# Chunks of tokens that never cross a batch edge, in an attention woven into a two-layer MLP kernel

## The reference

```python
k_p = k.reshape(B, H, 72, 8, D).mean(axis=3)
v_p = v.reshape(B, H, 72, 8, D).mean(axis=3)
scores = scale * np.matmul(q, k_p.transpose(0, 1, 3, 2))
scores = scores - np.max(scores, axis=-1, keepdims=True)
attn = np.exp(scores)
attn = attn / (np.sum(attn, axis=-1, keepdims=True) + 1e-09)
x = np.matmul(attn, v_p)                    # -> 4608 tokens x 512
# layer 1: h = x @ w_in; g = h if h >= 1, 0 if h <= -1, else (h + 1)**2 / 4; x = g @ w_out
# layer 2: h = x @ w_in; g = h - tanh(h);                                    x = g @ w_out
```

## Time and profile before

| | |
|---|---|
| median of 3 runs | 1709.42 us (1708.79 to 1709.98) |
| the profiled execution's own time | 1709.42 us |
| its span in the trace | 1707.7 us |
| PE busy | 1677.3 us, 98% |
| DVE / ACT / POOL busy | 768.4 / 496.2 / 183.9 us |
| mean DMA rate | 46 GB/s |

### The profile page before, as it was taken

How to read it: one execution, slowest core, us unless ns; L and a number is a source line. 1 busy time by engine, 2 the same in 40 slices (tenths; PEclk the granted TensorE clock), 3 DMA queues, 4 the chain that set the end, 5 groups by cost and what they waited for, 6 DMA issues and landing times.

```text
span 1707.7 us, 17885 instructions
## 1 busy us (share of the span) xinstructions
PE 1677.3 (98%) x7668; PEld 1392.3 (82%) x7668; DVE 768.4 (45%) x1197; ACT 496.2 (29%) x816; POOL 183.9 (11%) x133
## 2 busy tenths in 40 slices
PE   4999999999999999999999999999999999999998
PEld 3888888888888888888888888888888888888887
DVE  7666656575665647555443323222232323232322
ACT  3533232323333233232343222222222222222221
POOL 4730202020020202001044000000000000000000
PEclk8999999999999999999999999999999999999999
DMA  9102011110201121010223010101010101010000
GB/s 314 62 28 86 29 50 38 53 62 29 86 28 50 37 78 38 0 50 1 74 99 124 0 50 1 50 0 50 0 50 0 50 0 50 1 50 1 25 1 25
DMA packets 40208, 77.71 MB, mean 46 GB/s; under 512 B 3264, under 2 KB 3264, under 8 KB 40128
## 3 DMA queue, kind: packets, MB, share of 16 engines
q1 hardware_dynamic: 40128, 76.56, 13.3%
HBM read 57.67 MB, written 18.87 MB: 45 GB/s over the span
## 4 chain that ended last, share of the span: by engine, by line
PE 98%; POOL 1%; SPq 1%; DMA 0%; DVE 0%; issue 0%; ACT 0%; POOLq 0%
PE acc_ps L453 46%; PE h_ps L445 33%; PE att_ps L445 7%; PE score_ps L445 6%; PE score_ps L490 1%; PE att_ps L469 1%; PE score_ps L469 1%; PE att_ps L481 1%; PE att_ps L490 0%; PE score_ps L491 0%; SPq L284 0%; DMA v_raw<-v 0%; POOL v_raw L391 0%; POOL prob L413 0%; PE score_ps L481 0%; PE att_ps L491 0%
## 5 line engine op out<-in xcount | busy, mean ns | idle before, releaser
L453 PE MATMUL acc_ps<-g_hi,wout_hi 128*128 128x512 f32 x1152 | 454.2, 394 | 0.0
L453 PE MATMUL acc_ps<-g_hi,wout_lo 128*128 128x512 f32 x1152 | 449.0, 390 | 0.0
L453 PE MATMUL acc_ps<-g_lo,wout_hi 128*128 128x512 f32 x1152 | 448.8, 390 | 0.0
L445 PE MATMUL h_ps<-x_hi,win_hi 128*128 128x512 f32 x828 | 328.7, 397 | 1.4 <-DVE x_lo L816 1.4
L445 PE MATMUL h_ps<-x_hi,win_lo 128*128 128x512 f32 x828 | 322.9, 390 | 0.0
L445 PE MATMUL h_ps<-x_lo,win_hi 128*128 128x512 f32 x828 | 322.6, 390 | 0.0
L730 DVE TENSOR_TENSOR h_ps<-h_ps,bent 128x512 f32<-128x512 f32 x207 | 144.5, 698 | 272.1 <-ACT bent L603 206.1
L453 PEld LDWEIGHTS acc_ps<-g_hi,wout_lo 128*128 128x128 f32 x1152 | 216.2, 188 | 46.1
L453 PEld LDWEIGHTS acc_ps<-g_hi,wout_hi 128*128 128x128 f32 x1152 | 216.3, 188 | 43.9 <-issue 0.8
L453 PEld LDWEIGHTS acc_ps<-g_lo,wout_hi 128*128 128x128 f32 x1152 | 216.6, 188 | 43.4
L719 DVE TENSOR_TENSOR g_lo<-h_ps,g_hi 128x512 fp32r<-128x512 f32 x207 | 143.0, 691 | 125.6 <-ACT g_hi L607 124.9
(11 more groups left out here) (128 smaller groups left out, 1488.5 us busy)
## 6 DMA issues: line engine op xcount, KB each, us to landing
stage<-kT SPq DMA_DIRECT2D x16, 576.0 KB, 4.9
q_sb<-qT SPq DMA_DIRECT2D x9, 1024.0 KB, 5.1
x2T_scratch<-out_sb SPq DMA_DIRECT2D x9, 1024.0 KB, 4.1
x_lo<-x2T_scratch SPq DMA_DIRECT2D x9, 1024.0 KB, 7.3
yT<-out_sb SPq DMA_DIRECT2D x9, 1024.0 KB, 5.1
win_raw<-w_in SPq DMA_DIRECT2D x8, 1024.0 KB, 6.0
wout_raw<-w_out SPq DMA_DIRECT2D x8, 1024.0 KB, 7.8
stage<-v SPq DMA_DIRECT2D x7, 1024.0 KB, 5.8
```

The costliest lines, as they stand in the source:

```text
L445: last = nc.tensor.matmul(h_bank(j, layer), w[:, c, j * P:(j + 1) * P], x_[:, c, :], start=(c == 0 and i == 0), stop=(c == KT - 1 and i == 2))
L453: last = nc.tensor.matmul(acc_ps[:, m, :], w[:, j, m * P:(m + 1) * P], g[:, j % GRING, :], start=(j == 0 and i == 0), stop=(j == FT - 1 an ...
```

## The change

`chunks(n)` now returns a flat list of (first column, rows, batch). A chunk that the edge would cut becomes two chunks of 64 rows. So n = 1, 3, 5, 7 have five chunks, two of them with 64 rows, and ten units at steps 2 to 6; the other n have four chunks of 128 as before. Every half has its own scores (to PSUM rows 0 to 63), maximum, shift, exponential, sum, reciprocal, normalisation, and its own transposes in each turn, with 64 weight rows, 64 moving columns of the identity, and 64 columns of the output bank. `CHMAX` goes from 4 to 5, so `prob` and the arena are 576 words longer, only chunks from the second on can lie under `out_sb`, and the wait for the store moves from chunk 0 to chunk 1.

```diff
-CHMAX = T // P
+CHMAX = 5
...
     for c in range(T // P):
-        cut = min(max(edge - c * P, 0), P)
-        out.append([part for part in [(0, cut, n - 1), (cut, P - cut, n)] if part[1] > 0])
+        lo, hi = c * P, (c + 1) * P
+        if hi <= edge:
+            out.append((lo, P, n - 1))
+        elif lo >= edge:
+            out.append((lo, P, n))
+        else:
+            out.append((lo, edge - lo, n - 1))
+            out.append((edge, hi - edge, n))
...
-assert OUT_AT >= PROB_AT and ...
+assert OUT_AT >= PROB_AT + HEADS * KEYS and ...
...
             def scores(n, k):
                 c, g = divmod(k, GROUPS)
+                first, rows, b = chunks(n)[c]
...
-                for row, rows, b in chunks(n)[c]:
-                    for e in range(2):
-                        p = 2 * g + e
-                        last = nc.tensor.matmul(score_bank(n, k)[row:row + rows, e * 2 * KEYS:(e + 1) * 2 * KEYS],
-                                                q_sb[:, p, c * P + row:c * P + row + rows], k_diag[:, b % 2, p, :],
-                                                start=True, stop=True)
+                for e in range(2):
+                    p = 2 * g + e
+                    last = nc.tensor.matmul(score_bank(n, k)[0:rows, e * 2 * KEYS:(e + 1) * 2 * KEYS],
+                                            q_sb[:, p, first:first + rows], k_diag[:, b % 2, p, :], start=True, stop=True)
...
             def turn(n, i, bank):
-                for c in range(len(chunks(n))):
+                for c, (first, rows, b) in enumerate(chunks(n)):
                     if i == TAIL_TURN:
-                        cols = prob_tail[:, c, :]
+                        cols = prob_tail[0:rows, c, :]
...
-                    last = nc.tensor.transpose(bank[:, c * P:(c + 1) * P], cols, ident[:])
+                    last = nc.tensor.transpose(bank[:, first:first + rows], cols, ident[0:rows, 0:rows])
...
             def shift(n, c, g):
-                if n > 1 and c == 0 and g == 0:
+                rows = chunks(n)[c][1]
+                if n > 1 and c == 1 and g == 0:
```

More of the change, by code:

```diff
@@ L88 @@
 OUT_AT = ARENA - KT * T
-assert OUT_AT >= PROB_AT and Y_AT + 2 * KT * T <= BENT_AT and VRAW <= 2 * KT * T
+assert OUT_AT >= PROB_AT + HEADS * KEYS and Y_AT + 2 * KT * T <= BENT_AT and VRAW <= 2 * KT * T
 SCORE_SCALE = 1.0 / (DH ** 0.5) / POOL
@@ L401, in normalise @@
                 i = before(n) + c + 1
+                rows = chunks(n)[c][1]
                 pool.wait_ge(rcp_done, i)
[L403 to L406, removed]
+                tails = prob[0:rows, c].rearrange("p g k -> p (g k)").rearrange("p (a r) -> p a r", r=PAIR_ROWS)[:, :, P:]
+                second = row_rcp[0:rows, c, :].rearrange("p (a e) -> p a e", e=2)[:, :, 1]
+                shape = [rows, 2, PAIRS, TAIL]
+                nc.gpsimd.tensor_tensor(prob_tail[0:rows, c].rearrange("p (i a r) -> p i a r", i=2, a=PAIRS),
                                         tails.unsqueeze(1).to_broadcast(shape),
@@ L411, in normalise @@
                 pool.wait_ge(tail_done, i)
-                pr = prob[:, c].rearrange("p g (h k) -> p (g h) k", k=KEYS)
-                nc.gpsimd.tensor_tensor(pr, pr, row_rcp[:, c, :].unsqueeze(2).to_broadcast([P, HEADS, KEYS]),
+                pr = prob[0:rows, c].rearrange("p g (h k) -> p (g h) k", k=KEYS)
+                nc.gpsimd.tensor_tensor(pr, pr, row_rcp[0:rows, c, :].unsqueeze(2).to_broadcast([rows, HEADS, KEYS]),
                                         ALU.mult).then_inc(norm_done, 1)
@@ L465, in scores @@
                     pe.wait_ge(shift_done, GROUPS * before(n) + k - 1)
-                for row, rows, b in chunks(n)[c]:
-                    for e in range(2):
-                        p = 2 * g + e
-                        last = nc.tensor.matmul(score_bank(n, k)[row:row + rows, e * 2 * KEYS:(e + 1) * 2 * KEYS],
-                                                q_sb[:, p, c * P + row:c * P + row + rows], k_diag[:, b % 2, p, :],
-                                                start=True, stop=True)
+                for e in range(2):
+                    p = 2 * g + e
+                    last = nc.tensor.matmul(score_bank(n, k)[0:rows, e * 2 * KEYS:(e + 1) * 2 * KEYS],
+                                            q_sb[:, p, first:first + rows], k_diag[:, b % 2, p, :], start=True, stop=True)
                 last.then_inc(scores_done, 1)
             def turn(n, i, bank):
-                for c in range(len(chunks(n))):
+                for c, (first, rows, b) in enumerate(chunks(n)):
                     if i == TAIL_TURN:
-                        cols = prob_tail[:, c, :]
+                        cols = prob_tail[0:rows, c, :]
                     else:
                         k = PAIR_ROWS * pair_of(i)
-                        cols = prob[:, c].rearrange("p g k -> p (g k)")[:, k:k + P]
-                    last = nc.tensor.transpose(bank[:, c * P:(c + 1) * P], cols, ident[:])
+                        cols = prob[0:rows, c].rearrange("p g k -> p (g k)")[:, k:k + P]
+                    last = nc.tensor.transpose(bank[:, first:first + rows], cols, ident[0:rows, 0:rows])
                 last.then_inc(turned, 1)
@@ L620, in exponent @@
             def exponent(n, c, g):
+                rows = chunks(n)[c][1]
                 act.wait_ge(shift_done, GROUPS * (before(n) + c) + g + 1)
-                pr = prob[:, c, g, :]
+                pr = prob[0:rows, c, g, :]
                 nc.scalar.activation(pr, pr, ACT.Exp, scale=SCORE_SCALE).then_inc(exp_done, 1)
@@ L772, in find_max @@
             def find_max(n, c, g):
+                rows = chunks(n)[c][1]
                 dve.wait_ge(scores_done, GROUPS * (before(n) + c) + g + 1)
-                nc.vector.tensor_reduce(row_max[:, c, g, :], score_bank(n, GROUPS * c + g)[:, 0:HG * KEYS].rearrange(
+                nc.vector.tensor_reduce(row_max[0:rows, c, g, :], score_bank(n, GROUPS * c + g)[0:rows, 0:HG * KEYS].rearrange(
                     "p (h k) -> p h k", k=KEYS), AX_X, ALU.max).then_inc(max_done, 1)
             def shift(n, c, g):
-                if n > 1 and c == 0 and g == 0:
+                rows = chunks(n)[c][1]
@@ L780, in shift @@
+                if n > 1 and c == 1 and g == 0:
                     dve.wait_ge(out_stored, PRIME + 16 * (n - 1))
                 dve.wait_ge(max_done, GROUPS * (before(n) + c) + g + 1)
-                nc.vector.tensor_tensor(prob[:, c, g, :].rearrange("p (h k) -> p h k", k=KEYS),
-                                        score_bank(n, GROUPS * c + g)[:, 0:HG * KEYS].rearrange("p (h k) -> p h k", k=KEYS),
-                                        row_max[:, c, g, :].unsqueeze(2).to_broadcast([P, HG, KEYS]),
+                nc.vector.tensor_tensor(prob[0:rows, c, g, :].rearrange("p (h k) -> p h k", k=KEYS),
+                                        score_bank(n, GROUPS * c + g)[0:rows, 0:HG * KEYS].rearrange("p (h k) -> p h k", k=KEYS),
+                                        row_max[0:rows, c, g, :].unsqueeze(2).to_broadcast([rows, HG, KEYS]),
@@ L785, in shift @@
                                         ALU.subtract).then_inc(shift_done, 1)
             def sum_rows(n, c):
+                rows = chunks(n)[c][1]
                 dve.wait_ge(exp_done, GROUPS * (before(n) + c + 1))
-                nc.vector.tensor_reduce(row_sum[:, c, :], prob[:, c].rearrange("p g (h k) -> p (g h) k", k=KEYS),
+                nc.vector.tensor_reduce(row_sum[0:rows, c, :], prob[0:rows, c].rearrange("p g (h k) -> p (g h) k", k=KEYS),
                                         AX_X, ALU.add).then_inc(sum_done, 1)
@@ L792, in add_eps @@
             def add_eps(n, c):
+                rows = chunks(n)[c][1]
                 dve.wait_ge(sum_done, before(n) + c + 1)
-                nc.vector.tensor_scalar(row_sum[:, c, :], row_sum[:, c, :], 1e-9, None, ALU.add).then_inc(eps_done, 1)
+                nc.vector.tensor_scalar(row_sum[0:rows, c, :], row_sum[0:rows, c, :], 1e-9, None, ALU.add).then_inc(eps_done, 1)
             def invert(n, c):
+                rows = chunks(n)[c][1]
                 dve.wait_ge(eps_done, before(n) + c + 1)
-                nc.vector.reciprocal(row_rcp[:, c, :], row_sum[:, c, :]).then_inc(rcp_done, 1)
+                nc.vector.reciprocal(row_rcp[0:rows, c, :], row_sum[0:rows, c, :]).then_inc(rcp_done, 1)
```

## The result

The changed kernel takes 1728.97 us (median of 4 runs, 1727.46 to 1730.7), the kernel before 1709.25 (4 runs): a ratio of 1.0114, 95% interval 1.0103 to 1.0127. The forecast was 1729.3. The profiled execution took 1728.9 us.

The account below looks back on a forecast made before the run. TensorE (PE), 98% of the chain, was taken to bound the kernel. Scores 7.3, turns 8.4 and the block 0 wait 4.2 sum to 19.9 us, added to 1709.42: 1729.3 us, range 1719 to 1733.

Parts of the forecast that it names:

- Scores, +7.3: Score units of odd n: each of four lone-half units priced at 0.91 us like today's split unit, +7.3 us in all.
- Turns, +8.4: Transposes of odd n: form change plus half an extra record, 0.42 us a turn, 20 turns, +8.4 us.
- the 0.8 to 0.9: Sign in the later profile: an odd n's turn takes 0.8 to 0.9 us from product to product.
- the 0.37 taken over from the 64-column units: Turns: entering and leaving a 64-row form assumed to cost 0.37 us once per turn, as for 64-column score units.
- 0.48 a turn: Turns: alternative by the weight-load rule (columns, not rows), 0.48 us a turn, the sum 1.2 us more.
- The wait in block 0, +4.2: Block 0, step 8: place_v on DVE takes turns with POOL, delaying gate 10's low half; PE waits 4.2 us once.
- The clock, 0: Block 0: PE's clock stays up through the 4.2 us stand, nothing added; a fall would mean the prediction is wrong.
- the 3 us kept for the upper end: Block 0: 3 us allowed in the range's upper end for a short spell of slow PE clock.
- The claim that the extra DVE, ACT and POOL work of blocks 2, 4, 6 costs nothing: Blocks 2, 4, 6: the added instructions on these engines cost nothing; no other PE wait should appear.
- 1 (no form for 64 rows): Turns need no form change and cost 1.1 us (0 to 2.2): 1722.3 us; chance alone 0.22, with rival 2 0.07.
- 2 (no wait): Block 0: DVE runs place_v in one go or meets POOL elsewhere, no stall: 1725.1 us; chance alone 0.13.
- 3 (the pair costs it): Scores: the pair in two column positions costs 0.37, lone halves 0.54; turns nothing: +1.4, 1710.8 us; chance 0.06.

Follow-up runs that it names:

- the halves apart: Kernel before, second half of each split score unit issued three matmuls later, inside the next product: 1715.96 us, ratio 1.0039.
- the full forms: Changed kernel with place_v in step 7, half chunks (except the last of n = 7) computed with 128 columns and transposed with 128 rows: 1714.6 us, ratio 1.003.
- halved turns alone: Kernel before, only the transposes of the chunk with the edge done as two of 64 weight rows and 64 columns: 1715.06 us, ratio 1.0033.
- busy matmuls in the wait: Changed kernel with 18 unused matmuls behind the first turn of block 0, keeping PE busy: 1726.46 us, ratio 1.0099.
- late weights: Kernel before, POOL's last two weight subtractions of block 0 made to wait for the clip of step 8: 1713.63 us, ratio 1.0025.
- place_v in step 7: Changed kernel with place_v one step earlier, step 7 instead of 8: 1721.82 us, ratio 1.0075.
- one weight piece ahead: Changed kernel with weight piece 6 subtracted before the fifth chunk's POOL multiplications instead of behind them: 1722.79 us, ratio 1.008.

## Why the prediction was right, and where it was not

The total, 1729.3 against 1728.97, is closer than its terms by luck: two misses of opposite sign cancelled, 2.4 us too much in the turns and 2.7 us too little in the clock.

*Scores, +7.3.* Right. Four units at 0.90 where two stood at 0.91 make 1.8 us an odd n, 7.2 in all. That a lone half pays for the whole form and gains nothing from being half is shown by the halves apart, and that the form is the price by the full forms.

*Turns, +8.4.* Right in mechanism, too large in size: 0.30 us a turn, 6.0 in all. The 0.79 us from product to product lie just under the 0.8 to 0.9 that the prediction named as its sign. The step that was off was the 0.37 taken over from the 64-column units; the 64-row form costs 0.30 at most, and the extra record, for which I added half of 0.11, is inside it. The halved turns alone gave +6.0. The prediction's sum by the Trainium skill, page "TensorE: Matmul & The Clock Gate", section LDWEIGHTS, was 0.48 a turn. It was 0.30, but that does not speak against the rule, which bears only on the 0.11 of the extra record: 0.20 for the form and 0.10 for a record make 0.30 too. No run here decides it.

*The wait in block 0, +4.2.* Right: 4.3 us in PE's waits, on the low half that was forecast, from 110.1 to 114.5 where 110.6 to 114.8 was said, place_v's three instructions 10.5 us long where about 10 were said. The taking of turns was reproduced in the kernel before (3.0 expected, 3.1 measured), and the wait went away when only place_v was moved, and all but 1.0 us of it when only one weight piece was.

*The clock, 0.* Wrong, and the prediction had named the clock's fall in block 0 as a sign of being wrong; only the 3 us kept for the upper end covered it. I took from one stand in the prologue, at least 4.9 us long, that a stand of 4.2 would not lower the clock. It is no bound: that row shows a stand that was long enough, not one that was too short. The clock fell after about 2.9 us. The product behind the wait took 5.46 - 2.77 = 2.7 us more: busy matmuls in the wait took 2.5 us of it back, and 0.2 is the slow start behind a wait, which the prediction had not either.

Together 7.2 + 6.0 + 4.3 + 2.7 = 20.2, less 0.4 in the odd blocks and 0.3 in the prologue: 19.5, the difference of the spans. Why the odd blocks are 0.1 us shorter was not tried. The claim that the extra DVE, ACT and POOL work of blocks 2, 4, 6 costs nothing held: their +3.2 to +3.4 is the 1.8 of the scores and the 1.5 of five turns, and no wait of PE is there.

The rivals: 1 (no form for 64 rows) falls with the halved turns, 2 (no wait) with the trace, 3 (the pair costs it) with the halves apart. None of the versions tried beats the kernel before by more than its interval.

## What to carry to other kernels

Halving a tile does not halve its matmuls. On a full PE a score unit of 64 weight columns cost 0.90 us where a whole one cost 0.54, and two halves of 64 rows in a turn cost 0.30 more than the one record they replace. The way into a form and out of it was 0.2 to 0.4 us here, paid once for two halves that run side by side or one behind the other, and twice for halves a product apart. Padding to the full form, where the surplus is written over, took back 7.2 us; the padded kernel is still 5.5 us slower than the one before. A short instruction on an idle engine costs by what it pushes behind it: look which long one now starts when another engine needs SBUF, and how much slack the value behind that has. And a stand that was long enough to lower the clock says nothing about a shorter one.

## What the runs showed of the hardware that I had not expected

Two 64-column halves to PSUM rows 0 and 64 run side by side without being asked: 8 records in 0.65 us, 4 in 0.64.

In the changed kernel the clock fell while PE stood, after about 2.9 us, and stayed low until about 119.8. With the late weights PE stood for 3.1 us at a clock of 1.00, and the clock fell only 0.9 us after it had gone back to work; it was low for about 3.4 us, not 6.8. So busy matmuls behind a wait are no sign that it was harmless. What decides between the two was not tried.

The slow spell of the prologue is not the same in every run either: with place_v in step 7 the granted clock was 1.00 from 32 us on, in the changed kernel 0.50 from 32 to 36. Block 0 began at 48.6 us there and at 50.7 in the changed kernel, and the profiled execution took 1719.7 us where the median of that kernel's runs is 1721.8. That is why the terms above are read within the blocks, and not from the spans.

A DVE instruction with a single SBUF input of 8 elements, the addition of 1e-9, took 3.62 us in the run with one weight piece ahead: a POOL instruction had begun 1.0 us before it, and both ended at 101.6. In the changed kernel, with no POOL instruction beside it, it took 0.16.
